# A recurrent-attention and expert-layer kernel: raw weights in a ring of four pairs, later units' maxima in two levels

## What is computed

```python
m_new = np.maximum(f_gate[:, :, t] + m, i_gate[:, :, t])
f_stab, i_stab = np.exp(f_gate[:, :, t] + m - m_new), np.exp(i_gate[:, :, t] - m_new)
C = f_stab[..., None, None] * C + i_stab[..., None, None] * np.einsum('bhd,bhe->bhde', vt, kt)
n = f_stab[..., None] * n + i_stab[..., None] * kt
denom = np.maximum(np.abs(nq), 1.0)          # nq = n . q,  h_tilde = C q
y[:, :, t] = 1.0 / (1.0 + np.exp(-o_gate[:, :, t])) * h_tilde / denom
...
for e in range(4):
    out += p[:, e:e + 1] * (np.maximum(x @ w1[e], 0.0) @ w2[e])
```

## Time and profile before

| | us |
|---|---|
| median of three executions | 422.12 (421.67 to 425.3) |
| the profiled execution | 423.53 |
| its span, first to last instruction | 421.8 |
| TensorE busy | 412.9 (98%) |
| VectorE, ScalarE, GpSimd busy | 178.0, 166.0, 152.0 |
| granted TensorE clock, whole span | 1.00 |

### The profile page before, as it was taken

The page is one execution under the profiler, slowest core; times in us unless marked ns, Lnnn a source line. Parts: engine busy times, 40 slices in busy tenths (PEclk is TensorE's granted clock), DMA queues, the critical chain, the costliest instruction groups (busy, mean ns, idle before and its releaser), DMA issues.

```text
span 421.8 us, 6991 instructions
## 1 busy us (share of the span) xinstructions
PE 412.9 (98%) x2680; PEld 398.4 (94%) x2680; DVE 178.0 (42%) x364; ACT 166.0 (39%) x338; POOL 152.0 (36%) x188
## 2 busy tenths in 40 slices
PE   8799999899999999999999999999999999999997
PEld 8699989899999999999999999999999999999996
DVE  5684765655555556436233232323113123131142
ACT  6865679465253735424121441143211332111111
POOL 3566833793445855313010660056200355000000
PEclk9999999999999999999999999999999999999999
DMA  8889999599741677400000232013200010010010
GB/s 204 276 313 300 251 251 266 172 251 259 209 130 68 178 251 204 152 2 1 2 0 2 68 138 68 2 67 117 92 2 0 20 50 2 0 37 27 2 62 31
DMA packets 16868, 47.71 MB, mean 113 GB/s; under 512 B 2003, under 2 KB 8660, under 8 KB 15748
## 3 DMA queue, kind: packets, MB, share of 16 engines
q1 hardware_dynamic: 15972, 44.43, 36.0%
q10 hardware_dynamic: 864, 2.84, 1.9%
HBM read 45.18 MB, written 2.05 MB: 112 GB/s over the span
## 4 chain that ended last, share of the span: by engine, by line
PE 89%; DMA 4%; DVE 3%; ACT 1%; issue 1%; POOL 1%; SPq 1%; DVEq 0%; POOLq 0%; ACTq 0%
PE hid_ps L988 40%; PE acc_ps L1007 34%; PE out_ps L944 4%; PE score_ps L1007 3%; DMA w_raw<-in_w_b 3%; PE score_ps L903 2%; PE out_ps L951 2%; PE add_ps L924 1%; PE hid_ps L867 1%; DMA m_u<-y_acc 1%; PE acc_ps L988 1%; POOL w_lo L415 1%; ACT dec_w L510 1%; SPq L304 1%; DVE split_qk L688 0%
## 5 line engine op out<-in xcount | busy, mean ns | idle before, releaser
L747 DVE SCALAR_TENSOR_TENSOR h_lo<-hid_ps,h_hi 128x384 fp32r<-128x384 f32 (+2 forms) x120 | 67.9, 566 | 220.4 <-ACT h_hi L545 220.3
L545 ACT ACTIVATE h_hi<-hid_ps 128x384 fp32r<-128x384 f32 (+2 forms) x120 | 59.7, 497 | 233.5 <-PE hid_ps L988 233.0
L1007 PE MATMUL acc_ps<-w_hi,h_hi 128*128 128x320 f32 x352 | 110.3, 313 | 0.1
L1007 PE MATMUL acc_ps<-w_hi,h_lo 128*128 128x320 f32 x352 | 108.7, 309 | 0.0
L1007 PE MATMUL acc_ps<-w_lo,h_hi 128*128 128x320 f32 x352 | 108.4, 308 | 0.0
L988 PE MATMUL hid_ps<-xt_hi,w_hi 128*128 128x384 f32 (+2 forms) x360 | 104.1, 343 | 0.1
L988 PE MATMUL hid_ps<-xt_hi,w_lo 128*128 128x384 f32 (+2 forms) x360 | 103.8, 342 | 0.3 <-POOL w_lo L415 0.2
L415 POOL TENSOR_TENSOR w_lo<-w_raw,w_hi 128x384 fp32r<-128x384 f32 x56 | 59.8, 1071 | 114.3 <-ACT w_hi L531 114.3
L988 PEld LDWEIGHTS hid_ps<-xt_hi,w_lo 128*128 128x128 f32 x360 | 65.4, 188 | 4.8 <-POOL w_lo L415 0.7
L1007 PEld LDWEIGHTS acc_ps<-w_hi,h_hi 128*128 128x128 f32 x352 | 66.2, 188 | 1.6 <-DVE h_lo L747 0.3
L1007 PEld LDWEIGHTS acc_ps<-w_lo,h_hi 128*128 128x128 f32 x352 | 66.2, 188 | 1.3
(11 more groups left out here) (163 smaller groups left out, 368.3 us busy)
## 6 DMA issues: line engine op xcount, KB each, us to landing
w_raw<-in_w_b SPq DMA_DIRECT2D x25, 704.0 KB, 4.3
raw<-in_qk_s SPq DMA_DIRECT2D x8, 960.0 KB
g_all<-g_dram SPq DMA_DIRECT2D x10, 512.0 KB, 9.3
kv<-in_kv_n SPq DMA_DIRECT2D x12, 352.0 KB, 7.8
w_raw<-in_w_b ACTq DMA_DIRECT2D x3, 704.0 KB, 4.6
out_y<-y_acc SPq DMA_DIRECT2D x12, 160.0 KB, 1.8
carry<-g_dram SPq DMA_DIRECT2D x30, 60.0 KB
q_pack<-in_q_p SPq DMA_DIRECT2D x10, 180.0 KB, 9.6
```

The source lines that it names most:

```text
L545: nc.scalar.activation(h_hi[:, M % RING, 0:cols], hid_bank(M)[:, 0:cols], ACT.Relu).then_inc(hid_hi, 1)
L747: nc.vector.scalar_tensor_tensor(h_lo[:, M % RING, 0:cols], hid_bank(M)[:, 0:cols], 0.0, h_hi[:, M % RING, 0:cols].bitcast(fp32), ALU.max, ...
L1007: last = nc.tensor.matmul(acc_ps[t][:, 0:DM], x, w, start=(f == 0 and i == 0), stop=(f == NF - 1 and i == 2))
```

## The change

- `w_raw` has four pairs, so pair 3 is asked for without a wait and every later one a pair earlier. The SBUF space comes from gate rows (`fi_sb`, `m_sb`, the gate tiles) that now lie in the part of `y_acc` where the output gates of units 4 to 11 land later.
- The later units' maxima are made in two levels. VectorE scans each of the 80 unit rows by itself (maximum and sum, `local_maxima`); TensorE moves the row ends to 16 rows (`move_ends`, 4 products), VectorE scans over the chunks (`unit_starts`), TensorE moves the starts back to 80 rows (`move_starts`, 5 products), and one operation joins them (`unit_maxima`). The two long scans and the five DMAs go.
- `raw` and `q_pack` are loaded over 128 partitions instead of 120.
- The order of the loads on SyncE's and ScalarE's queues changes. `cast`, `subtract_high` and `reload_scores` stand one slot earlier. GpSimd's `mask_heads` moves ahead of `weigh_keys`, and the wait for the units' gates there goes.
- The sigmoid of the output gates becomes tanh of half the argument, plus one; the factor of two is taken up by the ones column (2.0) and the floor (2.0). The calls that switched tables go.

```diff
-RAW_PAIRS = 3
+RAW_PAIRS = 4
-OPEN_IN = {10: (4,), 13: (6, 8), 14: (10,)}
+OPEN_IN = {12: (4,), 13: (6, 8), 14: (10,)}
...
+        early = y_acc[0:U1, 4:NT, :].rearrange("u n m -> u (n m)")
...
+        local = row(4, U1, 2).rearrange("u (t l) -> u t l", t=2)
+        shift, m_u = early[0:U0, 6 * L:6 * L + 2 * U1 - U0], row(8, U1)
...
@@ SyncE
             sp.dma_start(fi_sb, fi_rows).then_inc(gates_in, 16)
+            sp.dma_start(fi_u[:, :, :], fi_units).then_inc(units_in, 16)
             load_scores(sp, 0)
...
-            for c in range(1, NC):
-                sp.wait_ge(m_half if c < 3 else m_ready, 1)
-                sp.dma_start(m_u[U0 * (c - 1):U0 * c, :], m_sb[:, L * c:L * (c + 1) + 1]).then_inc(m_moved, 16)
+            load_q(2)
+            reload_scores(2)
+            reload_scores(3)
             sp.wait_ge(gate_tiles[1]["ready"], 2)
             ...
-            reload_scores(2)
+            sp.wait_ge(out_done, 1)
+            sp.wait_ge(add_done, 1)
+            load_kv(sp, 2)
             sp.wait_ge(gate_tiles[1]["stored"], 3 * 16)
             load_g(2)
             load_carry(2)
-            load_q(2)
-            sp.wait_ge(out_done, 1)
-            sp.wait_ge(add_done, 1)
-            load_kv(sp, 2)
-            load_pair(sp, 3)
-            load_pair(sp, 4)
-            load_g(3)
-            load_carry(3)
-            reload_scores(3)
             load_q(3)
             sp.wait_ge(out_done, 2)
             sp.wait_ge(add_done, 2)
             load_kv(sp, 3)
+            load_pair(sp, 3)
+            load_g(3)
+            load_carry(3)
+            load_pair(sp, 4)
             load_pair(sp, 5)
+            load_pair(sp, 6)
+            load_pair(sp, 7)
+            reload_scores(4)
             sp.dma_start(y_acc[:, 4:NT, :], o_n[:, 4:NT, :]).then_inc(o_in[2], 16)
-            load_pair(sp, 6)
-            reload_scores(4)
-            load_pair(sp, 7)
...
-                if M == T0[3] + 5:
+                if M == T0[3] + 4:
                     reload_scores(5)
-                if (k := unit_at(M, -1)) is not None and NS <= k < NT - 2:
+                if (k := unit_at(M, -2)) is not None and NS <= k < NT - 2:
@@ ScalarE
-                nc.scalar.activation(o, o, ACT.Sigmoid).then_inc(open_ready, 1)
+                nc.scalar.activation(o, o, ACT.Tanh, scale=0.5).then_inc(open_ready, 1)
...
             decays(0, 0)
             decays(0, 1)
+            load_pair(act, 0)
             decays(1, 0)
             decays(1, 1)
             key_exp(0)
-            act.dma_start(y_acc[:, 2:4, :], o_n[:, 2:4, :]).then_inc(o_in[1], 16)
-            load_pair(act, 0)
-            act.dma_start(dp[:, :, :], dom_p).then_inc(dp_in, 16)
-            gate_open(2)
-            turn_table(ACT.Exp)
+            load_pair(act, 1)
             split_high(0, None)
-            load_pair(act, 1)
             load_pair(act, 2)
             split_high(1, None)
+            act.dma_start(y_acc[:, 2:4, :], o_n[:, 2:4, :]).then_inc(o_in[1], 16)
+            act.dma_start(dp[:, :, :], dom_p).then_inc(dp_in, 16)
+            xt_high(0)
+            xt_high(1)
             split_high(2, None)
             split_high(3, None)
-            xt_high(0)
-            xt_high(1)
+            gate_open(2)
@@ VectorE
+            def unit_steps():
+                gt = gate_tiles[1]
+                dve.wait_ge(m_ready, 1)
+                dve.wait_ge(local_ready, 3)
+                nc.vector.tensor_tensor(gt["fm"][:, :], gt["w"][:, :], m_u[:, :], ALU.add).then_inc(gt["step"], 1)
+                dve.wait_ge(gt["step"], 1)
+                nc.vector.tensor_scalar(gt["g"][:, :], gt["fm"][:, :], 0.0, None, ALU.min).then_inc(gt["step"], 1)
+                nc.vector.tensor_scalar(gt["j"][:, :], gt["fm"][:, :], 0.0, -1.0, ALU.max, ALU.mult)...
+            def local_maxima():
+                dve.wait_ge(units_in, 16)
+                nc.vector.tensor_tensor_scan(local[:, 0, :], fi_u[:, 0, :], fi_u[:, 1, :], NEG, ALU.add, ALU.max)...
+                nc.vector.tensor_tensor_scan(local[:, 1, :], ones[0:U1, 0:L], fi_u[:, 0, :], 0.0, ALU.mult, ALU.add)...
+                nc.vector.tensor_tensor(gate_tiles[1]["w"][:, :], fi_u[:, 0, :], fi_u[:, 1, :], ALU.subtract)...
+            def unit_starts():
+                dve.wait_ge(ends_ps, 1)
+                ends = hid_ps[0][0:U0, 0:2 * (NC - 2)].rearrange("u (c t) -> u c t", t=2)
+                nc.vector.tensor_copy(end_sums, ends[:, :, 1]).then_inc(ends_set, 1)
+                dve.wait_ge(ends_set, 1)
+                nc.vector.tensor_tensor_scan(m_sb[:, L + 1:L + NC - 1], end_sums, ends[:, :, 0], m_sb[:, L:L + 1], ...)
+            def unit_maxima():
+                dve.wait_ge(starts_ps, 1)
+                nc.vector.tensor_copy(m_u[:, 0:1], hid_ps[0][0:U1, U0:U0 + 1]).then_inc(m_begun, 1)
+                dve.wait_ge(m_begun, 1)
+                dve.wait_ge(local_ready, 2)
+                nc.vector.scalar_tensor_tensor(m_u[:, 1:L], local[:, 1, 0:L - 1], m_u[:, 0:1], local[:, 0, 0:L - 1], ...)
...
             probs(0, 0)
+            unit_maxima()
             probs(0, 1)
+            unit_steps()
             probs(1, 0)
-            dve.wait_ge(units_in, 16)
-            dve.wait_ge(m_moved, 16 * (NC - 1))
-            gate_steps(1, fi_u[:, 0, :], fi_u[:, 1, :], m_u[:, 0:L], m_u[:, 1:L + 1])
+            gate_scan(1)
             probs(1, 1)
             copy_keys(0, 0, U0, acc_ps[2])
-            gate_scan(1)
             gate_sums(1)
@@ TensorE
+            def move_ends():
+                pe.wait_ge(local_ready, 2)
+                for c in range(NC - 2):
+                    last = nc.tensor.matmul(hid_ps[0][0:U0, 2 * c:2 * c + 2], ident[0:U1, U0 * c:U0 * (c + 1)],
+                                            local[:, :, L - 1], start=True, stop=True)
+                last.then_inc(ends_ps, 1)
+            def move_starts():
+                pe.wait_ge(starts_ready, 1)
+                pe.wait_ge(shift_set, 2)
+                for c in range(NC - 1):
+                    at = U1 - U0 - U0 * c
+                    last = nc.tensor.matmul(hid_ps[0][0:U1, U0:U0 + 1], shift[:, at:at + U1], m_sb[:, L + c:L + c + 1], ...)
+                last.then_inc(starts_ps, 1)
...
             exponents_first(1, 1)
+            move_ends()
             scores(0, 0)
+            move_starts()
             scores(0, 1)
```

More of the change, by code:

```diff
@@ L134, in landing, with row @@
             return ctx.enter_context(nc.sbuf_tensor(name, shape, fp32, align_bytes=LINE))
-        fi_u, raw = landing("fi_u", [U1, 2, L]), landing("raw", [KS, 2, 2, H, L])
-        q_pack, carry = landing("q_pack", [KS, 2, GROUP, L]), landing("carry", [KS, 2, GROUP, L])
+        fi_u, raw = landing("fi_u", [U1, 2, L]), landing("raw", [128, 2, 2, H, L])
+        q_pack, carry = landing("q_pack", [128, 2, GROUP, L]), landing("carry", [KS, 2, GROUP, L])
         g_all, kv = landing("g_all", [L, 2, H, L]), landing("kv", [L, 2, KV])
         y_acc, w_raw = landing("y_acc", [L, NT, DM]), landing("w_raw", [128, 2 * RAW_PAIRS, WB])
-        m_u = sb("m_u", [U1, L + 1])
         state, fresh = sb("state", [KS, B, GROUP * GROUP * DA]), sb("fresh", [KS, GROUP * GROUP * DA])
+        early = y_acc[0:U1, 4:NT, :].rearrange("u n m -> u (n m)")
+        def row(at, rows, n=1):
+            return early[0:rows, at * L:(at + n) * L]
+        fi_sb = row(0, U0, 2).rearrange("u (g s) -> u g s", g=2)
+        m_sb, end_sums = early[0:U0, 2 * L:3 * L + NC], early[0:U0, 3 * L + NC:3 * L + 2 * NC - 2]
+        local = row(4, U1, 2).rearrange("u (t l) -> u t l", t=2)
+        shift, m_u = early[0:U0, 6 * L:6 * L + 2 * U1 - U0], row(8, U1)
         gate_tiles = []
-        for n, r in ((0, U0), (1, U1)):
+        for n, r, at in ((0, U0, 9), (1, U1, 12)):
             gate_tiles.append({
-                "fm": fresh[0:U0, 0:L] if n == 0 else sb("fm1", [r, L]),
-                "g": fresh[0:U0, L:2 * L] if n == 0 else sb("g1", [r, L]), "j": sb(f"j{n}", [r, L]),
-                "gg": sb(f"gg{n}", [r, 2, L]), "w": sb(f"w{n}", [r, L]), "key": sb(f"key_u{n}", [r, L]),
+                "fm": fresh[0:U0, 0:L] if n == 0 else row(18, r),
+                "g": fresh[0:U0, L:2 * L] if n == 0 else row(17, r), "j": row(at, r),
+                "gg": (sb("gg0", [U0, 2 * L])[:, :] if n == 0 else row(at + 3, r, 2)).rearrange("u (t l) -> u t l", t=2),
+                "w": row(at + 1, r), "key": row(at + 2, r),
                 "step": sem(f"gate_step{n}"), "ready": sem(f"g_ready{n}"), "exp": sem(f"gexp_ready{n}"),
@@ L231, in load_scores @@
             if k >= NS:
-                eng.dma_start(raw[:, kept(k), :, :, :], qk_s[k - NS]).then_inc(qk_in[kept(k)], 16)
+                eng.dma_start(apart[:, kept(k), 0:2 * H * L], qk_s[k - NS]).then_inc(qk_in[kept(k)], 16)
                 return
@@ L448, in _ @@
             count_weights(1)
-            pool.wait_ge(gate_tiles[1]["ready"], 2)
+            mask_heads()
             weigh_keys(0)
@@ L453, in _ @@
```

(17 more changed lines are left out.)

78 lines of the change are left out of this document (38 added, 40 removed).

## The result

The changed kernel takes 424.53 us, median of 20 executions (422.85 to 426.61), beside 422.5 us for the kernel before in the same session. The ratio is 1.0043, 95% interval [1.0027, 1.0058]: 1.8 us slower by the ratio, 2.0 by the medians, where 4.0 faster was forecast (418.1, range 416.8 to 420.6). The profiled execution has a span of 423.8 us against 421.8, so the profiles differ by 2.0, as the medians do.

A forecast was written before the change was run, and what follows sets the result against it. TensorE, busy 98% of the span, was taken as the bound, so only its idle time could be won. 0.9 + 1.5 + 1.7 - 0.1 = 4.0 us off 422.12 gave 418.1 us, range 416.8 to 420.6.

The forecast's parts named there:

- The maxima: Opening: two-level maxima remove VectorE's 2.29 us wait; `up(0)` starts at about 20.0 instead of 20.93, 0.9 us won.
- 0.06 a pass: Opening: estimated TensorE price of the 18 new passes that move the maxima, 1.1 us in all.
- rival D: `gate_open`: tanh and exp share no table, so table loads remain, one before `relu(0)`; about 2 us, 420.1; chance 0.04.
- I take pair 3 as 1 us earlier: Slot 4: pair 3, issued at about 22.7 against 23.73, lands 1 us earlier, so the opening's 0.9 survives.
- Rival A: Slot 4, `up(6)`: the opening's gain of 0.9 is eaten there; 3.1 us won, 419.0; chance 0.17.
- rival E: Pair 3 takes 18.4 us and lands at 41 where 29.2 is needed; 8 us lost after gains, 430; chance 0.03.
- The output gates of 2 and 3: Before `relu(0)`: their `gate_open` was mentioned only for possible table loads; their load got no term in the sum.
- Ring, +1.5: Around 56 to 60 us: four pairs and new load order bring pair 7 in the forties; 1.5 us of waits go.
- rows over 128 partitions: Score loads: 64 KB more per load, 0.3 us at 241 GB/s, behind transfers with slack; booked at 0.
- Casts, +1.7 - 0.1: At 80 us the wait before `scores(5, 0)` goes, 1.7 won; `relu(24)` late in slot 24 costs 0.1, bound 0.6.
- The profiled execution: Whole kernel: profiled 423.53 becomes 419.5; the same 4.0 us is taken off the median of 422.12.

The follow-up runs named there:

- e1: The changed kernel with the output gates of units 2 and 3 opened at the end of slot 2, not directly before `relu(0)`: 424.97 us, ratio 1.0057.
- e2: The changed kernel with q of unit 2 and scores of units 2 and 3 asked for after the three gate stores: 422.29 us, ratio 0.9983.
- e3: The changed kernel with the edits of both e1 and e2: 422.25 us, ratio 0.9986.
- e15: e3 with SyncE's loads of the scores and q of unit 3 moved behind pair 3 and unit 3's gates and carry: 421.70 us, ratio 0.9965.
- e10: e2 with the weight ring cut back from four pairs to three: 422.36 us, ratio 0.9989.
- e9: The kernel before, with only scores of units 4 and up and `q_pack` loaded over 128 rows instead of 120: 422.44 us, ratio 0.9984.
- e6: The kernel before, with only casts, their subtractions and the reload of the last scores one slot earlier: 422.43 us, ratio 0.9990.
- e13: e9 with casts, their subtractions and the reload of the last scores one slot earlier: 422.25 us, ratio 0.9994.

## Why the prediction was wrong, point by point

- *The maxima*: right. `up(0)` at 20.10 against 20.0. The ten passes took 0.87 with the tail, the eight 0.35; 0.06 a pass was near enough. No table load stands between 7 and 38 us on ScalarE: rival D did not come.
- *"I take pair 3 as 1 us earlier"*: the step that failed, and the one that decides, since in e1 the other loss was gone and the time stayed. Pair 3 was issued at 27.82 and not 22.7, and was there at 34.3, 3.9 us later than before and not 1 earlier. The text counted the 0.9 MB as running "while SyncE waits for gates" and did not ask what those bytes do to the stores that SyncE then waits for. The stores' price, 2.0 us in the kernel before, was taken for fixed; it was 6.6 here, and with the stores ahead of SyncE's loads (e2, e3) there was no wait left for them. The 0.9 MB cost a second time: with the stores first pair 3 was there at 31.4 (e2), still a microsecond later than before, and only with the scores and q of unit 3 behind it at 29.3 (e15). Rival A named the place and capped the loss at 0.9, and rival E had the price of a late pair (decides from a landing at 33.2; it landed at 34.3) and a chance of only 0.03. Both took a landing time from the old order of loads.
- *The output gates of 2 and 3*: not costed at all. The move of the load behind three pairs and of `gate_open(2)` ahead of `relu(0)` was seen under rival D, for its table load only. A step that moves past three loads of 704 KB on a queue and stands in front of the first `relu` has a landing of its own: 10.4 us from issue, 2.05 us on TensorE and 1.7 more by the clock. By e2 this too comes from SyncE's loads ahead of the stores.
- *Ring, +1.5*: a gain of 1.2 came, for another reason. Pair 7 was down by 43.8, as said; but e10 finds no worth in the fourth pair, and e9 has the gain from the step booked at 0, *rows over 128 partitions*. And e6, with 120 rows and three pairs, has more than half of that gain. The size came right by luck. The row that spoke was there: 241 GB/s at a full DMA share, beside 329 in the opening; the sum used it as a rate for all loads and never asked why it was low.
- *Casts, +1.7 - 0.1*: the 1.7 came in the trace; the price was 1.0 at 89 and 96, not 0.1 (bound 0.6), and by e13 against e9 another 0.7 at 56 to 60. `relu(24)` was mis-sized by half a us, and `q_pack`, on GpSimd beside `subtract_high`, was not in the sum.
- *The profiled execution*: the waits of one execution were priced and taken off the median. e13's trace has most of them gone, and its median has not moved. e6 has 0.9 of the 1.5 at 56 us gone though nothing was done for it. This is the second way in which 4.0 was too much: the best version here, e15, won 1.5.

The range (416.8 to 420.6) ended 4 us short of the measured time, because the most that it allowed for pair 3 was 0.9, for a load whose landing hung on a chain: bulk loads, stores, SyncE's wait, gates, pair.

## What to carry to other kernels

When a change moves loads forward, follow each small transfer that the same queue later waits for: bulk in front of it, on any queue, can move everything behind that wait. Put what is needed first in front, and a store that gates others ahead of the bulk. And read GB/s beside the DMA share: a full share at half the rate is a reason to ask for the shape of the load in flight. Last, take a wait of one profiled execution for a wait of that execution, until a second one has it too.
